# Windowed attention on one core: the eight global keys joined to the 96 keys before a tile, row sums taken from ones in the values, and all scores of a query tile in one run of matmuls

## What is computed

```python
scores = q @ k.T / sqrt(64)
is_global = pos_k < 8
is_local = (rel >= 0) & (rel < 96)            # rel = pos_q - pos_k
scores += -slope[h] * where(is_global & ~is_local, 96, abs(rel))
scores = where(is_global | is_local, scores, -1e9)
a = exp(scores - max)
x = (a / (sum(a) + 1e-9)) @ v                 # then two mixing layers on x
```

## Time and profile before

| | |
|---|---|
| median of 3 runs | 526.08 us |
| the profiled execution | 526.17 us, span 524.4 us |
| PE busy | 506.5 us (97%) |
| DVE busy | 267.0 us (51%) |
| ACT busy | 181.3 us (35%) |
| POOL busy | 139.9 us (27%) |
| granted TensorE clock | 1.00 |
| attention stage (0 to the first L270 at 106.37) | 106.37 us |
| moved by DMA | 35.02 MB |

### The profile page before, as it was taken

The page is one execution under the profiler, slowest core; times in us unless marked ns, Lnnn a source line. Parts: engine busy times, 40 slices in busy tenths (PEclk is TensorE's granted clock), DMA queues, the critical chain, the costliest instruction groups (busy, mean ns, idle before and its releaser), DMA issues.

```text
span 524.4 us, 8204 instructions
## 1 busy us (share of the span) xinstructions
PE 506.5 (97%) x3060; PEld 471.5 (90%) x3060; DVE 267.0 (51%) x671; ACT 181.3 (35%) x466; POOL 139.9 (27%) x129
## 2 busy tenths in 40 slices
PE   2999899999999999999999999999999999999997
PEld 2899789978999999988999999998888899888897
DVE  6999999645111321146211234337766574664452
ACT  4899899733111111122111133522232230321120
POOL 3556556159960000002200013550220130000040
PEclk9999999999999999999999999999999999999999
DMA  7755453405430000000300003230000011000002
GB/s 265 266 187 177 175 187 124 142 2 180 135 128 0 1 1 0 1 0 2 121 1 1 0 1 120 89 112 1 1 1 1 0 63 61 0 1 0 1 30 91
DMA packets 9257, 35.02 MB, mean 67 GB/s; under 512 B 1152, under 2 KB 3200, under 8 KB 7808
## 3 DMA queue, kind: packets, MB, share of 16 engines
q1 hardware_dynamic: 9216, 34.48, 19.2%
HBM read 31.33 MB, written 3.15 MB: 66 GB/s over the span
## 4 chain that ended last, share of the span: by engine, by line
PE 88%; DVE 6%; issue 3%; ACT 2%; DMA 1%; DVEq 0%; ACTq 0%
PE bank L270 70%; PE bank L1332 6%; PE bank L1115 5%; PE bank L1080 3%; PE bank L1096 2%; DVE scores L854 1%; PE bank L1188 1%; DVE wsplit L769 1%; PE bank L1215 1%; DVE wsplit L780 1%; ACT probs L624 1%; PE bank L1143 1%; ACT probsT L578 1%; DMA counts<-both_counts 1%; DVE bias L847 0%
## 5 line engine op out<-in xcount | busy, mean ns | idle before, releaser
L270 PE MATMUL bank<-hid,wsplit 128*128 128x384 f32 (+1 forms) x648 | 126.4, 344 | 0.1
L270 PEld LDWEIGHTS bank<-hid,wsplit 128*128 128x128 f32 x648 | 113.3, 188 | 3.9 <-issue 0.7
L270 PE MATMUL bank<-split,wsplit 128*128 128x384 f32 x576 | 108.1, 337 | 0.0
L270 PE MATMUL bank<-wsplit,zs 128*128 128x512 f32 (+1 forms) x576 | 104.1, 340 | 0.0
L270 PEld LDWEIGHTS bank<-wsplit,zs 128*128 128x128 f32 x576 | 89.1, 188 | 13.3
L270 PEld LDWEIGHTS bank<-split,wsplit 128*128 128x128 f32 x576 | 100.3, 188 | 0.0
L989 DVE SCALAR_TENSOR_TENSOR hid<-bank,hid 128x384 fp32r<-128x384 f32 x48 | 26.7, 557 | 140.4 <-ACT hid L703 140.4
L556 POOL TENSOR_TENSOR wsplit<-wraw,wsplit 128x1536 fp32r<-128x1536 f32 (+1 forms) x18 | 58.6, 3261 | 75.3 <-ACT wsplit L664 74.4
L703 ACT ACTIVATE hid<-bank 128x384 fp32r<-128x384 f32 x48 | 23.6, 491 | 144.0 <-PE bank L270 144.0
L555 POOL CAST wsplit<-wraw 128x1536 fp32r<-128x1536 f32 (+1 forms) x12 | 15.9, 1324 | 129.2 <-PE bank L270 123.1
L624 ACT ACTIVATE probs<-scores,nmax 128x232 f32<-128x232 f32 (+1 forms) x96 | 44.7, 467 | 10.5 <-DVE nmax L854 9.9
(11 more groups left out here) (103 smaller groups left out, 534.4 us busy)
## 6 DMA issues: line engine op xcount, KB each, us to landing
wraw<-weights SPq DMA_DIRECT2D x16, 768.0 KB, 4.0
qk_raw<-qk SPq DMA_DIRECT2D x11, 1056.0 KB, 4.9
vt<-v SPq DMA_DIRECT2D x12, 256.0 KB, 3.3
out<-act_raw SPq DMA_DIRECT2D x16, 192.0 KB, 1.9
wraw<-weights SPq DMA_DIRECT2D x4, 512.0 KB, 3.4
qk_raw<-qk SPq DMA_DIRECT2D x1, 792.0 KB, 5.2
vg<-v_first SPq DMA_DIRECT2D x2, 256.0 KB, 5.4
qk_raw<-qk SPq DMA_DIRECT2D x1, 264.0 KB, 3.5
```

Source lines behind the costliest of these rows:

```text
L270: mm = pe.matmul(dst, lhs(a), rhs(c), start=first and i == 0, stop=last and i == 2, skip_group_check=True)
```

## The change

- **Keys joined.** The window of a tile becomes [96 keys before | 8 global keys] (104 together, `SEEN`) and the own 128. One transpose takes all 128 queries against the 104, one the own tile, both 128 columns wide. The values come with a second block in which the host has put the 96 rows before and the 8 first rows (`vt[..., 1, :]`). L1133, L1143, L786, L595, L803, L602 and L808 go, with `vg`, `gprobs`, the load of `v_first` and the clearing of unused probabilities on POOL. In tile 0 the global keys are in the own block, so its scores have 128 columns instead of 136, and their bias is folded into the own one by a maximum.
- **Sums from ones.** Each head's values get a 65th column of ones. The product's column 64 is the sum; the exponentials lose their accumulators. An output bank holds 4 heads (260 columns), so a unit is finished in two halves q: `read_sums`, `invert_sums`, `take_x` on 256 columns, at odd steps m with q = (m-5)//2.
- **Scores in one go.** PE issues the scores of all 4 pairs of a unit at the unit's first step, each pair into a bank of its own (two heads side by side). `keys_lo` and `queries_hi` run one step further ahead (m+4, m+5), as does `keys_hi`.
- **Start.** DVE first writes 1.0 into a free block, and PE runs 9 matmuls of 512 columns on it. The low part of the first unit's queries moves from DVE to POOL, where it stands ahead of the flag's small operations. ACT makes 6 of the 8 biases, DVE 2.
- **Buffers.** `vt` has 2 places instead of 3 and its load waits `pv_done`; a load is 520 KB for tiles 1 to 5 and 260 KB for tile 0. Borrowed slots start at 5 instead of 4.

The diff, cut to its core:

```diff
-PROBS_AT = 2
+PROBS_AT = 3
-BORROWED = 4
+BORROWED = 5
...
+        def scores_at(m, e):
+            n, p = divmod(m, PAIRS)
+            first = UNSEEN if n % T else OWN
+            return S_BANK[p][:, e * (WIN - UNSEEN) + first - UNSEEN:(e + 1) * (WIN - UNSEEN)]
...
-                if n >= 3:
-                    sp.wait_ge(o_ready, n - 1)
-                sp.dma_start(vt[:, n % 3], v[b, t]).then_inc(v_in[n % 3], 16)
+                if n >= 2:
+                    sp.wait_ge(pv_done, PAIRS * (n - 1))
+                blocks = slice(0, 2 if t else 1)
+                sp.dma_start(vt[:, n % 2, blocks], v[b, t, :, blocks]).then_inc(v_in[n % 2], 16)
...
                         act.activation(probs[:, n % 2, h, first:], scores[:, m % 2, e, first:], ACT.Exp,
-                                       bias=nmax[:, n % 2, h:h + 1], scale=-1.0,
-                                       accum_out=psum[:, n % 2, h:h + 1]).then_inc(exp_done, 1)
+                                       bias=nmax[:, n % 2, h:h + 1], scale=-1.0).then_inc(exp_done, 1)
...
+            def read_sums(q):
+                dve.wait_ge(pv_done, 2 * (q + 1))
+                if q >= 2:
+                    dve.wait_ge(x_done, q - 1)
+                dve.tensor_scalar(rinv[:, q % 2].unsqueeze(2), weighed(q)[:, :, D:], 1.0e-9, None,
+                                  ALU.add).then_inc(sums_ready, 1)
...
                 if m == 0:
-                    for later in range(2, PAIRS):
-                        split_first(later)
...
+                    split_first(1)
+                    split_first(2)
+                if m == 1:
+                    split_first(3)
+                    queries_hi(1, 0)
+                    queries_hi(1, 1)
+                    keys_lo(1, 0)
+                q = (m - 5) // 2 if m >= 5 and m % 2 else None
+                if q is not None:
+                    read_sums(q)
+                if m and m + PAIRS + 1 < STEPS:
+                    queries_hi(*divmod(m + PAIRS + 1, PAIRS))
+                if q is not None:
+                    invert_sums(q)
+                if m and m + PAIRS < STEPS:
+                    keys_lo(*divmod(m + PAIRS, PAIRS))
+                if q is not None:
+                    take_x(q)
...
-                if m >= 2:
-                    pe.wait_ge(ttr_done, 2 * (m - 1))
+                if m >= PAIRS:
+                    pe.wait_ge(ttr_done, 2 * (m - PAIRS + 1))
...
+            pe.wait_ge(ones_ready, 1)
+            for i in range(WARM):
+                pe.matmul(PT_BANK[i % 2][:, :], w_at(TOK1, 0, 0, P), w_at(TOK1, 0, 0, 512))
...
-                if m < STEPS:
-                    head_scores(m)
-                if p == 2 and n >= 1:
-                    pe.wait_ge(gathered, n)
...
+                if m < STEPS and p == 0:
+                    for ahead in range(PAIRS):
+                        head_scores(m + ahead)
```

More of the change, by code:

```diff
@@ L75, with build @@
 PI_IN = 3.1415925
[L78 removed]
+def build(nc, qk, v, both_counts, weights, out):
     ctx = ExitStack()
@@ L184, in build @@
         qk_in = [sem(f"qk_in{i}") for i in range(2)]
-        v_in = [sem(f"v_in{i}") for i in range(3)]
+        v_in = [sem(f"v_in{i}") for i in range(2)]
         k_hi = sem("k_hi")
@@ L613, in _ @@
                     flag = load_flag(act)
-                if n >= 1 and p == 2:
-                    global_probsT(n - 1)
                 if m < STEPS:
-                    first = UNSEEN if n % T else P
+                    first = UNSEEN if n % T else OWN
                     for e in range(2):
@@ new lines, in read_sums, with invert_sums, take_x @@
+            def read_sums(q):
[4 more added lines that the diff above has]
+                                  ALU.add).then_inc(sums_ready, 1)
+            def invert_sums(q):
+                dve.wait_ge(sums_ready, q + 1)
+                dve.reciprocal(rinv[:, q % 2], rinv[:, q % 2]).then_inc(rinv_ready, 1)
+            def take_x(q):
+                b, half = divmod(q, 2 * T)
+                dve.wait_ge(rinv_ready, q + 1)
+                dve.tensor_tensor(act_raw[:, b, half * HALF_H * D:(half + 1) * HALF_H * D].rearrange(
+                                      "p (h d) -> p h d", h=HALF_H),
+                                  weighed(q)[:, :, 0:D],
+                                  rinv[:, q % 2].unsqueeze(2).to_broadcast([P, HALF_H, D]),
+                                  ALU.mult).then_inc(x_done, 1)
@@ L826, in split_first @@
                 keys_lo(0, p)
-                heads = slice(2 * p, 2 * p + 2)
-                dve.wait_ge(q_hi, p + 1)
-                dve.tensor_tensor(q_split[D:P, 0, heads], q_in[D:P, 0, heads],
-                                  q_split[D:P, 0, heads].bitcast(F32), ALU.subtract).then_inc(q_lo, 1)
             split_first(0)
-            for h in range(H // 2):
+            for h in range(2):
                 dve.tensor_scalar(bias[:, h, :], c_base, SLOPES[h], None, ALU.mult).then_inc(bias_ready, 1)
             build_global_bias()
-            split_first(1)
+            dve.wait_ge(bias_ready, H)
+            link(dve.tensor_copy(own_bias[:, :, :], bias[:, :, OWN:OWN + G]))
             for m in range(STEPS):
@@ L858, in _ @@
                                              accum_out=nmax[:, n % 2, h:h + 1]).then_inc(ttr_done, 1)
-                if p == 1 and n >= 1:
-                    gather(n - 1)
                 if m == 0:
-                    for later in range(2, PAIRS):
-                        split_first(later)
-                if n + 1 < UNITS:
-                    queries_hi(n + 1, p)
-                if 1 <= m <= STEPS - PAIRS:
-                    keys_lo((m - 1) // PAIRS + 1, (m - 1) % PAIRS)
-                if p == 2 and n >= 1:
-                    global_probsT_lo(n - 1)
-                    invert_sums(n - 1)
-                if p == 0 and n >= 2:
-                    take_x(n - 2)
-                if p == 1 and n % T == 1:
-                    global_values_lo(n // T)
-            take_x(UNITS - 2)
-            gather(UNITS - 1)
-            global_probsT_lo(UNITS - 1)
-            invert_sums(UNITS - 1)
-            take_x(UNITS - 1)
+                    split_first(1)
[16 more added lines that the diff above has]
+                    take_x(q)
+            for q in range(2 * UNITS - 2, 2 * UNITS):
+                read_sums(q)
+                invert_sums(q)
+                take_x(q)
             general_vector(dve, flag)
-            dve.wait_ge(x_done, UNITS)
+            dve.wait_ge(x_done, 2 * UNITS)
             def rows_at(ap, s):
@@ L1069, in head_scores @@
                 if place == 0:
-                    first, key = P, 0
+                    first, key = OWN, G
                 else:
@@ L1091, in transpose_probs @@
                 for e in range(2):
-                    for i in range(2):
-                        if i == 0 and n % T == 0:
-                            continue
-                        at, queries = e * PT_HEAD + i * REACH, (REACH, P)[i]
-                        mm = pe.transpose(PT_BANK[m % 2][:, at:at + queries],
-                                          probs[0:queries, n % 2, m % PAIRS * 2 + e, i * OWN:i * OWN + P],
-                                          ident[0:queries, 0:queries])
+                    h, at = m % PAIRS * 2 + e, e * PT_HEAD
+                    if n % T:
+                        pe.transpose(PT_BANK[m % 2][0:SEEN, at:at + P], probs[:, n % 2, h, UNSEEN:OWN],
+                                     ident[:, :])
+                    mm = pe.transpose(PT_BANK[m % 2][:, at + P:at + 2 * P], probs[:, n % 2, h, OWN:],
+                                      ident[:, :])
                 mm.then_inc(pT_ready, 1)
@@ L1375 @@
     first_keys = np.broadcast_to(kc[:, 0:1, :, :, 0:G], (B, T, D, H, G))
-    v_first = np.zeros((B, 2, H, G, H, D), v.dtype)
-    for h in range(H):
-        v_first[:, :, h, :, h] = v[:, None, h, 0:G]
+    rows = np.concatenate([v, np.ones((B, H, S, 1), v.dtype)], axis=3)
+    rows = rows.transpose(0, 2, 1, 3).reshape(B, T, P, H * VD)
+    v_rows = np.zeros((B, T, P, 2, H * VD), v.dtype)
+    v_rows[:, :, :, 0] = rows
+    v_rows[:, 1:, 0:REACH, 1] = rows[:, :-1, UNSEEN:]
+    v_rows[:, 1:, REACH:SEEN, 1] = rows[:, 0:1, 0:G]
     def tiles(w):
```

205 lines of the change are left out of this document (78 added, 127 removed).

## The result

The changed kernel takes 522.28 us (median of 5 runs, 521.70 to 524.35), the kernel before 526.11 (5 runs): a ratio of 0.9936, interval 0.9922 to 0.9951. That is 3.8 us faster; the forecast was 7.3, 518.8. The sign held and the size was half. The time lies inside the wide range, 513.5 to 525.0, and 0.3 above the forecast's own, 516 to 522.

What follows compares the result with a forecast made beforehand. PE was taken to bound attention at 6.84 us a unit. Start 24.5, unit 11's scores at 88.0, attention's end at 99.1 instead of 106.37: 7.3 less, 518.8 us; own range 516 to 522, wide 513.5 to 525.0.

Steps and rivals of the forecast that it cites:

- PE, 6.84 a full unit: PE in attention: four steps of 1.71 us make 6.84 a full unit, from 7.17, and set the pace.
- ACT 6.2: ACT in a full attention unit: exponentials, copies and keys take 6.2 us, no longer near the bound.
- I add nothing: Scores in one go: ACT lacking copies and scores needing DVE's reductions cost 0 extra, while DVE stays inside its slack.
- DVE 5.96 and a stall of 0.85: DVE in a full unit: 5.96 us of work, plus 0.85 waiting for values at the second step, 6.8 in all.
- rival 3: DVE's `keys_lo` loses the race with POOL every time, 7.9 to 8.5 us a unit, total 531.0; chance 0.10.
- hidden, with 1 to 1.5 us to spare: Loads of queries and keys issued 6.8 us before use, landing in 4.9, so costing nothing.
- Start: Unit 2's load issued at 12.2 us, PE starting its scores at 24.5 instead of 25.46: a gain of 1.0.
- Constant matmuls: Nine matmuls at the start: nothing left of them at 16 us; if the clock stayed, 2.0 us less.
- Rival 1: Clock holds and DVE swallows all disturbances: 2.0 and 3.2 us less, total 513.6; chance 0.13.
- From unit 2 to 11: Attention between these units' scores: eight full units 54.7 us, unit 6 5.6 bound by DVE, disturbances 3.2.
- rival 2: DVE sets the pace: `keys_lo` loses to POOL now and then, 7.4 us a unit, total 523.3; chance 0.12.
- rival 4: PE waits for DVE at score runs; a unit stays at 7.6 us, only start and end gain, 524.2; chance 0.10.

Runs made afterwards that it cites:

- Experiments 2 and 3: Changed kernel with the joined block resized: 128 or 96 keys (k128 523.98, k96 522.89 us), then 96 or 104 queries (q96 523.29, cut 523.93 us).
- c64: Changed kernel with products taking 64 columns of values instead of 65, sums read from column 63 (no true weights): 522.91 us, ratio 0.9934 to the kernel before.
- k128: Changed kernel with the joined block padded from 104 to 128 keys by 24 cleared columns: 523.98 us, ratio 0.9948 to the kernel before.
- k96: Changed kernel with 96 keys in the joined block instead of 104, 8 local keys of each tile left out: 522.89 us, ratio 0.9925 to the kernel before.
- q96: Changed kernel with the joined block transposed and weighed for the first 96 queries only: 523.29 us, ratio 0.9926 to the kernel before.
- cut: Changed kernel with global keys swapped with the own block's first 8, so the joined block serves 104 queries, output whole: 523.93 us, ratio 0.9942 to the kernel before.
- cuthalf: Changed kernel with the changes of cut and halves together, output whole: 521.99 us, ratio 0.9936 to the kernel before.
- vhalf: Changed kernel loading only the values' own block from the fourth unit on, output differs: 522.75 us, ratio 0.9929 to the kernel before.
- halves: Changed kernel with each unit's load of queries and keys issued in two halves of four heads: 521.64 us, ratio 0.9904 to the kernel before.
- warm2: Changed kernel with 2 constant matmuls at the start instead of 9: 522.62 us, ratio 0.9923 to the kernel before.
- fill: Changed kernel with 28, 2, 14 and 2 filler transposes behind the first unit's pairs of scores: 522.20 us, ratio 0.9926 to the kernel before.
- steps: Changed kernel with each pair's scores issued in its own step again: 525.70 us, median of seven; ratio 0.9969 to the kernel before, without two runs of 555.
- best: Changed kernel with moved global keys, loads in halves and filler transposes together, output whole: 521.41 us, ratio 0.9907 to the kernel before.
- after: The changed kernel itself, with no further edit, in its profiled execution of 524.35 us; its median is 522.28 us.

## Why the forecast was half right

- **PE, 6.84 a full unit; measured 7.18.** This is the step that failed. "In tile 0, where all do, four take 0.37, so eight take 0.74": the first two of such a group start 0.06 apart and each later one 0.11, so doubling counted the short first distance twice. Eight take 0.84, and 0.20 more once a unit where the first products wait: 4 x 0.10 + 0.20 too little. The scores in one go take 1.87 (32.86 to 34.73) instead of 4 x 0.53: 0.25 too much. The difference, 0.35, is the 0.34 that a unit lacks. The 0.84 also lies above the 0.70 to 0.80 that the prediction gave as bounds. Against the kernel before, L1133, L1143 and the run gave 0.69 + 0.25, and the transposes (4 x 0.05), the values (4 x 0.14) and the wait (0.20) took 0.96: nothing was left of the gain in a unit. Experiments 2 and 3 show that the 32 more queries of the joined block made its instructions longer: 0.15 of a step's 1.28.
- **Column 65 and the 104 rows cost nothing:** right (c64, k128, k96).
- **ACT 6.2:** right, 12.61 in two units. "I add nothing" for the run of scores was 0.20 a unit too little at 7.18, the wait of the last products for ACT's copy (L581), and more below: at 7.03 to 7.07 ACT holds PE (q96, cut, cuthalf).
- **DVE 5.96 and a stall of 0.85:** the sums were right in their parts (`read_sums` 0.08, reciprocal 0.09, `take_x` 0.33). The stall at L777 was 0.7 us in two full units (33.05 to 47.42) instead of 0.85 in each, and 8.1 in ten waits from 26 to 105 us. Casts that meet POOL slices were priced in rival 3 only: DVE is busy for 13.43 in two units, not 11.9.
- **Loads "hidden, with 1 to 1.5 us to spare":** wrong. They landed in 6.1 and stood in the chain for 26.6%, in this profile. vhalf and halves had none of it there, for no gain that vhalf's median shows and 0.6 us in that of halves.
- **Start:** unit 2's load went out at 13.37 (12.2 forecast), because POOL's fourth subtraction ended only then, and its scores at 25.68 (24.5). No gain of 1.0, a loss of 0.2.
- **Constant matmuls:** right, and by the run, not only by the argument (warm2). By the rule of the Trainium skill (TensorE: Matmul & The Clock Gate, section HAM oscillation) they would buy nothing; the trace agrees, 0.63 for the first four and 3.89 for the run at 16.74. Rival 1's 2.0 us for a clock that holds were wrong too: with the clock held (fill) the third unit started only 0.5 earlier.
- **From unit 2 to 11:** 65.7 us measured, 63.5 forecast. Eight full units at 7.18 are 2.7 more; unit 6 took 6.15, not 5.6, and was bound by PE (busy 6.15 of 6.15, its run of scores 1.81 long, hardly less than a full unit's 1.87), not by DVE (4.74); disturbances took 2.1, not 3.2. So the error in PE is a little larger than the sum shows, and another hid 1.1 of it. **The end:** 11.6 and 11.1. **Behind it:** 1.5 of clock in the profiled run, not in the forecast.

Added up: start 1.2, units 2.2, end 0.5, handover 1.5, which makes 5.4 for the profiled run of 524.35 (forecast 518.9). The median is 2.1 shorter; for the other four runs no profile divides the time.

Rivals 2 and 3 did not come: `keys_lo` started ahead of POOL in odd steps too (0.41). That rival 2's 523.3 lies near the measured time is chance. Nor did rival 4: a full unit took 7.18, not 7.6, and its run of scores has no gap; its 524.2 is near by chance too. The contention of VectorE and GpSimd that the Trainium skill (GPSIMD Engine Reference, section Specifications) describes showed at another instruction, the cast at 37.87. The page names VectorE instructions with two SBUF inputs or in a 2-port mode; the cast has one input, and whether it runs in such a mode no run here shows. Having two inputs was not enough to slow `keys_lo`: it had started first.

## What to carry to other kernels

Before you join two small blocks, ask which of their sizes is paid for: here the number of queries, not of keys, so that a block with fewer queries was cheap and the joined one was not. Take the cost of a group from the distance of its later members, not from a short group doubled. And when three engines are this near each other (busy for 14.37, 13.43 and 12.61 us of two units' 14.37), a cut on one shows mostly as the next bound: put a number on the second and third before you sum.

## What was not expected of the hardware

- A joined fp32 transpose or product took 0.085 us with 96 queries, 0.09 with 104 and 0.11 with 128, with 96, 104 or 128 keys alike, and products of 64, 65 or 66 moving columns took the same. In products the queries are the columns of weights, in transposes the columns that move.
- TensorE can stay at half its pace for some 90 us of nearly gapless work: in the profiled one of the two long runs of steps PE was busy in 83 of 89 us, and yet a step took 3.39 instead of 1.78 until 95 us, with a granted clock of 1.00 in the record.
- Half-clock stretches of 3.4 to 13.7 us began in unit 6 at 56 to 57 us (k96, q96, cut, warm2), near 68 us, in unit 8 (c64, halves, best), or at the handover (after, k128, q96), in some runs of a kernel and not in others.
